# Loading 112 instead of 128 partitions of the transposed k and r tiles

## The reference, cut to what matters

```python
batch, n_heads, seq, head_dim = (2, 8, 768, 48)

def _attn_ref(r, k, v, w, u):
    state = np.zeros((B, H, D, D))
    for t in range(S):
        kt, vt, rt = (k[:, :, t], v[:, :, t], r[:, :, t])
        cur = np.einsum('bhd,bhe->bhde', u[None] * kt, vt)
        y[:, :, t] = np.einsum('bhd,bhde->bhe', rt, state + cur)
        state = w[None, :, :, None] * state + np.einsum('bhd,bhe->bhde', kt, vt)

def reference(**kwargs):
    attn_out = _attn_ref(**attn_kwargs)           # (2, 8, 768, 48)
    x = attn_out.transpose(0, 2, 1, 3).reshape(B * S, H * D)   # 1536 rows of 384
    x = _moe_ref(x=x, **moe_kwargs)               # top 1 of 8 experts, 384 -> 1024 -> 384
    return _moe2_ref(x=x, **moe2_kwargs)          # the same with a capacity of 384 rows
```

## Time and profile before

| | |
|---|---|
| median of 3 runs | 387.48 us |
| lowest, highest | 386.71, 388.46 us |
| profiled execution, its own time | 388.46 us |
| its span in the profile | 386.7 us |
| mean granted clock of TensorE | 0.966 |
| busy share PE, DVE, ACT, POOL | 93%, 53%, 35%, 43% |
| DMA moved | 68.41 MB, mean 177 GB/s |
| krT loads | 12 of 512 KB, median 6.7 us from issue to landing |

### The profile page before, as it was taken

How to read it: one execution, slowest core, us unless ns; L and a number is a source line. 1 busy time by engine, 2 the same in 40 slices (tenths; PEclk the granted TensorE clock), 3 DMA queues, 4 the chain that set the end, 5 groups by cost and what they waited for, 6 DMA issues and landing times.

```text
span 386.7 us, 10327 instructions
## 1 busy us (share of the span) xinstructions
PE 361.5 (93%) x3266; PEld 349.9 (90%) x3267; DVE 206.0 (53%) x538; ACT 136.5 (35%) x284; POOL 165.0 (43%) x290
## 2 busy tenths in 40 slices
PE   5899999889899999999999999789999999999990
PEld 5788888778899999999999998679999999999990
DVE  3756666587788555555555585655115555144110
ACT  1456666412455222211222252114225555255120
POOL 4778886034555333333333252344423434344311
PEclk9669999989999999999999999899999999999996
DMA  7967786168999211111111502059269987592100
GB/s 238 411 225 255 275 295 232 63 189 282 390 388 395 93 41 41 41 41 41 41 41 41 191 18 45 11 176 376 68 216 356 336 310 255 180 341 71 30 21 17
DMA packets 31616, 68.41 MB, mean 177 GB/s; under 512 B 5669, under 2 KB 21332, under 8 KB 31456
## 3 DMA queue, kind: packets, MB, share of 16 engines
q1 hardware_dynamic: 27696, 57.56, 42.0%
q0 software_dynamic: 3744, 10.23, 8.2%
q10 hardware_dynamic: 144, 0.20, 0.5%
HBM read 59.15 MB, written 10.14 MB: 179 GB/s over the span
## 4 chain that ended last, share of the span: by engine, by line
PE 86%; DMA 5%; DVE 3%; issue 1%; ACT 1%; POOL 0%; SPq 0%; ACTq 0%; DVEq 0%; POOLq 0%
PE p_h L1241 36%; PE p_o L1263 28%; PE p_sc L1153 4%; PE p_y L1140 4%; PE p_x L1117 4%; DMA w_sb<-in_moe_w 3%; PE p_y L1128 3%; PE p_xt L1218 2%; PE p_kv L1108 2%; DMA w_col<-in_w_by_dim 1%; PE p_o L1084 1%; DMA xg<-x_rows,src_idx 1%; PE p_sl L1185 1%; PE p_x L1084 1%; DVE grow L819 0%
## 5 line engine op out<-in xcount | busy, mean ns | idle before, releaser
L1241 PE MATMUL p_h<-xT,w_sb 128*128 128x128 f32 x1296 | 149.3, 275 | 2.3 <-DMA w_sb<-in_moe_w 1.3
L1241 PEld LDWEIGHTS p_h<-xT,w_sb 128*128 128x128 f32 x1296 | 148.3, 192 | 3.0 <-DMA w_sb<-in_moe_w 1.7
L1016 DVE SCALAR_TENSOR_TENSOR h_lo<-p_h,h_hi 128x512 fp32r<-128x512 f32 x54 | 37.3, 692 | 79.8 <-ACT h_hi L778 78.7
L1033 DVE CUSTOM_DVE_ANT_0 lg_prod<-y_row,wg_all 128x384 f32<-128x384 f32 x112 | 55.7, 553 | 41.7 <-ACT y_row L788 41.6
L1263 PE MATMUL p_o<-w_hi,h_hi 128*128 x216 | 75.2, 348 | 0.0
L1263 PE MATMUL p_o<-w_hi,h_lo 128*128 x216 | 73.0, 338 | 0.0
L1263 PE MATMUL p_o<-w_lo,h_hi 128*128 x216 | 73.0, 338 | 0.0
L778 ACT ACTIVATE h_hi<-p_h 128x512 fp32r<-128x512 f32 x54 | 32.3, 598 | 112.9 <-PE p_h L1241 105.2
L586 POOL TENSOR_TENSOR dst_mark<-zeros 128x1 f32<-128x1 f32 x54 | 14.2, 263 | 107.0 <-DVE y_row L1033 67.6
L864 DVE TENSOR_TENSOR w_lo<-w_raw,w_hi 128x1024 fp32r<-128x1024 f32 x36 | 42.0, 1221 | 7.7 <-ACT w_hi L676 7.0
L1263 PEld LDWEIGHTS p_o<-w_lo,h_hi 128*128 128x128 f32 x216 | 40.7, 188 | 0.0
(11 more groups left out here) (179 smaller groups left out, 380.2 us busy)
## 6 DMA issues: line engine op xcount, KB each, us to landing
w_raw<-in_moe_w SPq DMA_DIRECT2D x12, 1536.0 KB
w_sb<-in_moe_w SPq DMA_DIRECT2D x12, 1536.0 KB
nat<-in_rkv SPq DMA_DIRECT2D x11, 576.0 KB, 5.6
krT<-in_kr_by_dim SPq DMA_DIRECT2D x12, 512.0 KB, 6.7
x_rows<-x_rows SPq DMA_DIRECT2D x12, 192.0 KB, 2.2
out<-zeros SPq DMA_DIRECT2D x1, 2304.0 KB
wg_all<-in_moe_w_gate_by_expert SPq DMA_DIRECT2D x1, 1536.0 KB, 7.8
xg<-x_rows,src_now POOLq DMA_INDIRECT x27, 3.1
```

Source lines behind the costliest of these rows:

```text
L1016: stt(h_lo[:, at, :], p_h[n][:, :, :], 0.0, h_hi[:, at, :].bitcast(F32), ALU.max, ALU.subtract).then_inc(h_ready[layer], 1)
L1033: last = nv.tensor_tensor_reduce(out=lg_prod[:, n, :], in0=y_row[par][:, 0:DM], in1=wg2_all[:, e, :], op0=ALU.mult, op1=ALU.add, scale=1.0 ...
L1241: last = mm(p_h[half][:, f, :], w1_sb[place][:, c, col:col + P], xT[:, c, :], start=(c == 0), stop=(c == DC - 1))
```

## The change

The host array `kr_by_dim` keeps rows 0 to 111 of each block (HD + D = 112), and the load writes partitions 0:R of the krT buffer. Partitions 112 to 127 of krT are then never written. The rest of the program is the same.

```diff
@@ load_krT
                 b, c, q = n % B, n // B, n % TRING
                 wait_pos(sp, kT_ready, n - TRING + 1)
                 wait_pos(sp, rT_ready, n - TRING + 1)
-                sp.dma_start(krT[q][:, :, :, :], kr_t[b, c, :, :, :, :]).then_inc(krT_loaded[q], 16)
+                sp.dma_start(krT[q][0:R, :, :, :], kr_t[b, c, :, :, :, :]).then_inc(krT_loaded[q], 16)
@@ laid_out
     rows = np.arange(HD) % D
     kr = np.stack([k, r]).reshape(2, B, H // 2, 2, S // T, T, D).transpose(1, 4, 3, 6, 0, 2, 5)
-    laid["kr_by_dim"] = kr[:, :, :, rows].reshape(B, S // T, 2 * HD, 2, H // 2, T)
+    laid["kr_by_dim"] = kr[:, :, :, rows].reshape(B, S // T, 2 * HD, 2, H // 2, T)[:, :, 0:HD + D]
```

## The result

The changed kernel took 388.75 us (median of 20 runs, 386.97 to 393.82) against 386.45 us before (20 runs in the same session): ratio 1.0056, 95% interval 1.0042 to 1.0070. It is slower by 2.3 us. The forecast was 387.4 us and no change. 388.75 lies in the stated range of 386.0 to 389.2, but by luck: the range was laid around the 387.48 of three runs, and the median of 20 runs of the same kernel is 1.0 us lower. Laid around 386.45, it would end at 388.2.

A forecast was written before the change was run, and what follows sets the result against it. TensorE was taken to bound the kernel, with 86% of the chain. All four terms (first load, second, ten others, weights) were 0; from the median of 387.48 us, half the first load's bound gave 387.4 us, range 386.0 to 389.2.

The forecast's parts named there:

- What bounds the kernel: Whole kernel: TensorE holds 86% of the chain, all DMA 5%; the start's chain begins with w_col, no krT load in it.
- Less traffic: All twelve krT loads: 64 KB less each saves 0.16 us a load, 1.9 us of transfer in all, beside compute.
- The issue and the shape: Loads on 112 partitions, absent from the trace: rate per byte taken to stay, each load 0.16 us shorter.
- my slow end: The other bound for a krT load on 112 partitions: half the rate, 2.24 us for 1.28, 0.96 us longer.
- The first load: First krT load at the start: 0.16 us sooner, all hidden from TensorE; price 0, between 0 and -0.16 us.
- the second load: Second krT load, read by L828: lands 0.3 us sooner, L828 stays behind L877 and the mask behind ACT; price 0.
- The ten others: The later krT loads: issued some three units of work ahead of their readers while TensorE is busy; price 0.
- What follows on the queue: Expert 0's w2 and w1 loads, behind krT on the queue: cover over 12 us, next stage not reached; price 0.
- Rival 1: Half-rate load delays the second landing, L828, mask and second score: +1.6 to +3.5 us, middle 390.0 us; chance 0.09.
- Its clock part: With longer idle at TensorE's second wait, the clock may rise one unit of work later, 1.9 us a unit.
- Rival 2: At the start, less TensorE idle lets the clock rise a unit earlier: 1.9 us faster, 385.4 us; chance 0.08.
- Rival 3: The krT loads are not shorter, since ports or latency bind, not bytes; landings stay, 387.5 us; chance 0.23.

The follow-up runs named there:

- b0_again: The kernel before, unchanged, run once more for a second profile: 385.23 us, one run, against 388.46 us in the first profile.
- The streams: Kernels holding only loads, attention and experts left out, output zeros, twelve loads a stream: kr alone 1.24 us a load on 128 partitions, 1.59 on 112.
- the order on VectorE: The changed kernel with kT and rT of unit 1 made behind the mask of unit 0 and the bonus of unit 1: ratio 1.0068 to before.

## Why the prediction was wrong

*What bounds the kernel.* Right in the main. The start has the thin places, and the 0.15 us at rT and 0.34 us at the second kT that it named are those that gave way. That no krT load is on the chain was true of the one profile that it had; in b0_again the first is.

*Less traffic.* The bytes fell by 0.79 MB (68.41 to 67.62 MB), as said. That they cost nothing and bring nothing when the rate holds is shown by the same bytes on 128 partitions.

*The issue and the shape.* This is the step that failed. It bounded an operation that the trace did not have by "the rate per byte stays" and "half the rate", and took the first, "as the loads of 128 partitions with rows of 4 and 4.5 KB beside it all move at about 409 GB/s". But those rows vary the row's length and hold the partitions fixed. They say nothing of a load that names fewer partitions. The streams show 1.59 us for 1.24 alone, and a pair 1.94 us longer (4.58 for 2.64), twice the 0.96 us that my slow end allowed. That end slowed only the load itself; it left out that the loads of nat in between slow down with it.

*The first load, the second load.* Priced at 0 each. They landed 1.3 and 3.0 us late, and the second score moved by 2.65 us. *The ten others*: 0 was right for the last eight when the first four come in time. It was not for krT 2: once the second is moved out of the way, the third score waits for it, as the order on VectorE showed.

*What follows on the queue.* Right: w2 of expert 0 was not waited for.

*The rivals.* Rival 1 is what happened, in its place and by its path: second load, L828, mask, second score. It said 13.9 for the second landing and +1.6 us before the clock; it was 15.0 and +2.65. I gave it 0.09, on the ground that 4 KB rows remained. Its clock part, a unit more at half speed, didn't occur in the pair of profiles, whose distance is the same 2.5 us at the third score and at the end. Between the profiles of the two kernels with more warm-up it put 2.9 us on top of the 2.0 to 2.3 of the loads. So the clock isn't the cause, but it can add to it. Rival 2 did not occur as an effect of the change; as scatter of one kernel it did, at 2.5 us a unit where I had 1.9. Rival 3 had the load "not shorter"; it was longer.

*The pages.* The Trainium skill (SBUF — State Buffer, "Door 1: The DMA port swizzle") has 0 to 63 on half of the ports. The stream on 64 partitions agrees, 205 GB/s for 421. What I worked out from it, 1.28 us for 112 partitions, was too low: 1.59 measured. The same page of the Trainium skill has a rule that I should have weighed as a rival of its own ("The DMA setup-cost knee"), to use 128 partitions where a transfer binds; the traces agree with it in every stream of twelve. The Trainium skill (DMA: Bandwidth & Descriptors, "Why a DMA increments its semaphore by 16 and not by 1") has a rule for the number of engines that gives 16 for 112 rows. The 16 packets of 4 bytes for each load agree, as do 15 for each load on 120 partitions, and it does not help. An account that fits is that seven rows to an engine no longer fall together with the groups of partitions that share a port, so that engines meet at ports, and more so when some of them are still at a load on 128. That is an inference: it fits packets of the same size that take longer, each by its own measure (183 to 259 ns for the middle eight tenths on 112, 159 for nearly all on 128), the dependence on place (1.47 and 1.59 us), the cost of taking turns, and the DRAM to DRAM copies. No run shows a port, and how HWDGE deals 112 rows to its engines stays open.

No version here that computes the whole result beats the kernel before. Trimming only the later loads equals it, and there is nothing to be won where TensorE works without a gap.

## What to carry to other kernels

Padding partitions of a load are not waste to be trimmed without a measurement: with rows of 4 KB on SP's full queue, naming 112 of 128 partitions made each load slower, not shorter, and slowed the full loads that took turns with it. Where bytes must go, shorter rows on 128 partitions kept the rate (2.5 us for 2.64 a pair). And when the trace holds no instance of an operation's new shape, a row that varies another dimension does not bound it; look for one that varies the same, or give the bad end the weight that the thin covers of the start deserve.

## What the runs showed of the hardware

A load on 64 partitions took as long as one on 128 with twice the bytes (1.28 and 1.24 us); its packets of 4 KB took a median of 331 ns each for 159. Loads on 112 and 128 partitions in turn took 4.58 us a pair where the first alone took 1.59 and nat, beside others on 128, about 1.40; in these turns the packets of nat took a median of 309 ns for 178. The 2 KB load of w_col, first in the queue, landed after 5.0, 3.2 and 4.3 us in three profiles with nothing changed ahead of it. TensorE's clock rose at 20.3 or at 25.5 us in two executions of one kernel, which put 2.5 us between them.
